# Bucketed attention before two feed-forward layers: sign bits placed under the features of the second score product, scores kept under a ceiling, and copies and loads in another order

## What is computed

```python
q_bits = einsum('bhsd,dk->bhsk', q, proj) > 0          # six bits a token
k_bits = einsum('bhsd,dk->bhsk', k, proj) > 0
mask = bucket(q_bits)[:, :, :, None] == bucket(k_bits)[:, :, None, :]
scores = where(mask, scale * q @ k.T, -1e9)
attn = exp(scores - max(scores)); attn /= attn.sum() + 1e-9
x = (attn @ v), heads laid side by side                # 1536 x 512
x = elu(x @ moe_w_in) @ moe_w_out                      # 512 -> 2048 -> 512
out = (s * relu(x @ moe2_w_in)**2 + b) @ moe2_w_out    # 512 -> 2048 -> 512
```

## Time and profile before

| | us |
|---|---|
| three runs | 781.66, 784.97, 785.71 (median 784.97) |
| the profiled execution | 782.37 |
| its span | 780.6 |
| PE busy (matmul) | 763.5 (98%), 3800 instructions |
| PEld busy (weight loads) | 644.7 (83%) |
| DVE busy (VectorE) | 405.1 (52%) |
| ACT busy (ScalarE) | 343.6 (44%) |
| POOL busy (GpSimd) | 288.9 (37%) |

### The profile page before, as it was taken

One profiled execution on the slowest core, in us unless ns is written; L12 is line 12 of the kernel. 1 busy time (PEld: TensorE's weight loads), 2 busy tenths in 40 slices (PEclk: granted clock), 3 DMA queues, 4 the chain that ended last, 5 costly groups with the idle time before them and its releaser, 6 DMA issues.

```text
span 780.6 us, 12163 instructions
## 1 busy us (share of the span) xinstructions
PE 763.5 (98%) x3800; PEld 644.7 (83%) x3800; DVE 405.1 (52%) x688; ACT 343.6 (44%) x657; POOL 288.9 (37%) x230
## 2 busy tenths in 40 slices
PE   7999999999999999999999999999999999999998
PEld 6788888888889888888888888888888888888886
DVE  5888887888898574343333432352323333242333
ACT  7988898888987221232212322132221312222121
POOL 3688878878897493000000366660000000000000
PEclk9999999999999999999999999999999999999999
DMA  6576667666762342000000032310001000010001
GB/s 168 136 148 167 146 141 177 151 127 157 157 120 61 84 136 82 1 0 1 1 0 1 27 100 89 107 55 0 1 1 42 11 0 0 0 54 0 0 0 54
DMA packets 46312, 52.77 MB, mean 68 GB/s; under 512 B 8912, under 2 KB 34768, under 8 KB 46288
## 3 DMA queue, kind: packets, MB, share of 16 engines
q1 hardware_dynamic: 46064, 52.13, 27.0%
q10 hardware_dynamic: 224, 0.33, 0.2%
HBM read 32.73 MB, written 3.19 MB: 46 GB/s over the span
## 4 chain that ended last, share of the span: by engine, by line
PE 75%; DMA 8%; POOL 6%; issue 5%; SPq 3%; DVE 2%; ACT 0%; POOLq 0%; DVEq 0%
PE acc L594 33%; PE h_ps L576 32%; DMA inv_dram<-row_inv 4%; DMA all_inv<-inv_dram 3%; PE pt_ps L542 2%; POOL wa_lo L431 2%; POOL kt L385 2%; PE pv_ps L556 2%; PE pv_ps L557 1%; PE s_ps L528 1%; PE s_ps L529 1%; POOL wa_hi L429 1%; POOL pt_hi L395 1%; DMA w_raw<-w_out_dram 1%; DVE w_raw L837 1%
## 5 line engine op out<-in xcount | busy, mean ns | idle before, releaser
L770 ACT ACTIVATE r_sb<-h_ps 128x512 f32<-128x512 f32 x96 | 57.4, 598 | 368.0 <-PE h_ps L576 368.0
L909 DVE TENSOR_SCALAR g_sb<-e_sb,sb_scale 128x512 f32<-128x512 f32 x48 | 27.9, 582 | 158.2 <-ACT e_sb L773 158.2
L907 DVE SCALAR_TENSOR_TENSOR g_sb<-e_sb,h_ps 128x512 f32<-128x512 f32 x48 | 33.0, 687 | 135.6 <-ACT e_sb L773 135.1
L804 DVE TENSOR_REDUCE row_min<-s_ps 128x1 f32<-128x768 f32 x96 | 91.5, 954 | 10.3 <-PE s_ps L529 9.6
L693 ACT ACTIVATE probs<-s_ps,row_min 128x768 f32<-128x768 f32 x96 | 87.0, 906 | 11.3 <-DVE row_min L804 9.3
L542 PE MATMUL pt_ps<-cst,probs 128*128 128x128 f32 x576 | 80.8, 275 | 0.7 <-DVE pt_lo L811 0.5
L556 PE MATMUL pv_ps<-pt_hi,v_nat 128*128 128x384 f32 x192 | 72.6, 378 | 7.8 <-DVE w_raw L837 7.7
L576 PE MATMUL h_ps<-xt_hi,wa_lo 128*128 (+1 forms) x192 | 74.7, 389 | 0.0
L576 PE MATMUL h_ps<-xt_lo,wa_hi 128*128 (+1 forms) x192 | 74.7, 389 | 0.0
L576 PE MATMUL h_ps<-xt_hi,wa_hi 128*128 (+1 forms) x192 | 74.7, 389 | 0.0
L576 PE MATMUL h_ps<-xt_hi,wb_hi 128*128 (+1 forms) x192 | 74.7, 389 | 0.0
(11 more groups left out here) (93 smaller groups left out, 1598.3 us busy)
## 6 DMA issues: line engine op xcount, KB each, us to landing
qt<-kt SPq DMA_DIRECT2D x45, 192.0 KB, 3.0
w_raw<-w_in_dram SPq DMA_DIRECT2D x32, 256.0 KB, 2.7
w_raw<-w_out_dram SPq DMA_DIRECT2D x32, 256.0 KB, 2.9
all_inv<-inv_dram SPq DMA_DIRECT2D x32, 192.0 KB, 3.7
raw<-qk_dram SPq DMA_DIRECT2D x15, 384.0 KB, 4.3
raw_v<-v_dram SPq DMA_DIRECT2D x16, 192.0 KB, 4.7
out_dram<-o_sb SPq DMA_DIRECT2D x12, 256.0 KB, 2.1
kt<-kt SPq DMA_DIRECT2D x15, 192.0 KB, 3.7
```

What stands on the lines that cost most here:

```text
L804: nc.vector.tensor_reduce(row_min[:, k:k + 1], s_ps[k % 2][:, :, 0:HALF], AX.XY, ALU.min).then_inc(min_done, 1)
```

## The change

The mask moves into 12 rows under the 64 features of the second product. For each of six bits there is a row for "bit set" and one for "bit clear"; q's rows hold +2^31 for its own side, k's rows -2^31 for the other, so each differing bit adds -2^62 to q·k. VectorE writes scores times -SCALE, under a ceiling of 2^56, to SBUF and takes the row's minimum in the same instruction; the exponential works in place there. The product of counts, the one-hot, the penalty and the scaling of q fall away. All sign products of a head stand in unit 5, the bits are written in unit 0 and one DMA lays them under q and k.

In `scores`, `exp` and the keeping of scores:

```diff
-                wait(pe, exp_done, u - 1)
+                wait(pe, scores_kept, u - 1)
-                q2 = qt2[par][:, t * P:(t + 1) * P]
+                q2 = qt2[par][score_rows, t * P:(t + 1) * P]
...
-                    last = mm(s_ps[buf][:, n, 0:HALF], q2, kt2[par][:, cols], start=False, stop=True)
+                    last = mm(s_ps[buf][:, n, 0:HALF], q2, kt2[par][score_rows, cols], start=False, stop=True)
...
-            def row_minimum(u, k):
+            def keep_scores(u, k):
                 dve.wait_ge(scores_done, u + 1)
-                nc.vector.tensor_reduce(row_min[:, k:k + 1], s_ps[k % 2][:, :, 0:HALF], AX.XY,
-                                        ALU.min).then_inc(min_done, 1)
+                wait(dve, pt_done, 2 * u - 2 * (SRING - 1))
+                ts(probs[k % SRING][:].rearrange("p (n c) -> p n c", n=2), s_ps[k % 2][:, :, 0:HALF], -SCALE, CEILING,
+                   ALU.mult, ALU.min, accum_out=row_min[:, k:k + 1]).then_inc(scores_kept, 1)
...
-                act.wait_ge(min_done, u + 1)
-                wait(act, pt_done, 2 * u - 2)
-                nc.scalar.activation(probs[k % 2][:].rearrange("p (n c) -> p n c", n=2), s_ps[k % 2][:, :, 0:HALF],
-                                     ACT.Exp, bias=row_min[:, k:k + 1], scale=-1.0,
-                                     accum_out=row_sum[:, k, 0:1]).then_inc(exp_done, 1)
+                act.wait_ge(scores_kept, u + 1)
+                scores = probs[k % SRING]
+                nc.scalar.activation(scores[:], scores[:], ACT.Exp, bias=row_min[:, k:k + 1], scale=-1.0,
+                                     accum_out=row_sum[:, k:k + 1]).then_inc(exp_done, 1)
```

Bits, the copies of q and of the bits, and the move of x of second heads (SRING is 3; `bit_rows` are partitions 64 to 75, `score_rows` 0 to 75; the sign products now give 48 rows):

```diff
+            def to_bits(dst, z, rows, thr, amp):
+                return ts(dst, z, planes_in_sb[rows, thr:thr + 1], planes_in_sb[rows, amp:amp + 1], ALU.is_gt, ALU.mult)
+
+            def copy_q_hi(head, par):
+                sp.wait_ge(qk_hi, head)
+                sp.dma_start(qqk[par][top, 0:2, :].bitcast(F32),
+                             hi.unsqueeze(1).to_broadcast([DH, 2, SEQ])).then_inc(q_hi_copied, 16)
...
+            def copy_bits(head, par):
+                sp.wait_ge(bits_done, head)
+                sp.nop(nofuse=True)
+                sp.wait_ge(q_lo_copied, 16 * head)
+                sp.dma_start(qqk[par][bit_rows, 1:3, :].bitcast(F32), bits[:].bitcast(F32)).then_inc(bits_copied, 16)
...
-                sp.dma_start(x_other[n][low, :], x_second[top, :]).then_inc(second_moved[n], 16)
-                sp.dma_start(x_main[n][low, :], x_second[low, :]).then_inc(second_moved[n], 16)
+                sp.dma_start(x_parts[n][low, :, :], x_second[n][:]).then_inc(second_moved[n], 16)
```

`x_second` becomes two buffers, `raw_v` two, x no longer lies in a weight buffer; the parts of v of odd heads are written interleaved, every second column. The order of SP's queue in a pair:

```diff
                 copy_k(2 * i + 1, 1)
+                copy_bits(2 * i + 1, 1)
                 if prev:
+                    get_inv(i, -1)
                     move_second(i - 1, 0)
-                    get_inv(i, -1)
+                if nxt:
+                    load_qk(2 * i + 3, 1)
+                    load_v(2 * i + 2, 0)
                 put_inv(i, 0)
-                load_v(2 * i + 1)
+                get_inv(i, 0)
                 if nxt:
-                    copy_q(2 * i + 2, 0)
+                    copy_q_hi(2 * i + 2, 0)
                 if prev:
                     move_second(i - 1, 1)
-                get_inv(i, 0)
-                if after:
-                    load_qk(2 * i + 4, 0)
                 if nxt:
-                    load_w(0, i + 1, 0, i + 1)
+                    copy_q_lo(2 * i + 2, 0)
                 put_inv(i, 1)
                 if nxt:
                     copy_k(2 * i + 2, 0)
+                    copy_bits(2 * i + 2, 0)
+                get_inv(i, 1)
                 move_first(i, 0)
-                get_inv(i, 1)
+                if after:
+                    load_qk(2 * i + 4, 0)
                 put_inv(i, 2)
...
```

GpSimd adds the epsilon (`add_eps`) and splits weights only in the first and the last pair (EARLY is 4 in place of 8; the other twelve tiles are split beside the first chunk):

```diff
-            def pair(i, prev=True, nxt=True):
+            def pair(i, prev=True, nxt=True, weights=()):
                 split_third(i, 0)
-                split_w(at(wa_hi, i), at(wa_lo, i), i, 0, i + 1)
+                add_eps(i, 0)
+                if weights:
+                    split_w(at(wa_hi, weights[0]), at(wa_lo, weights[0]), weights[0], 0, weights[0] // 2 + 1)
+                if prev:
+                    split_x(i - 1, 0)
                 if nxt:
                     split_qk(2 * i + 2, 0)
+                add_eps(i, 1)
                 split_third(i, 1)
                 if prev:
-                    split_x(i - 1, 0)
+                    split_x(i - 1, 1)
                 split_third(i, 2)
-                split_v(2 * i + 1, 1)
-                if prev:
-                    split_x(i - 1, 1)
+                add_eps(i, 2)
+                split_v(2 * i + 1, 1, i + 1)
+                if weights:
+                    split_w(at(wa_hi, weights[1]), at(wa_lo, weights[1]), weights[1], 1, weights[1] // 2 + 1)
                 if nxt:
                     split_qk(2 * i + 3, 1)
+                add_eps(i, 3)
                 split_third(i, 3)
```

More of the change, by code:

```diff
@@ L461, in _ @@
             split_qk(1, 1)
[L462 to L463 removed]
+            split_v(0, 0, 1)
+            pair(0, prev=False, weights=(0, 1))
             with pool.Fori(1, PAIRS - 1) as i:
                 pair(i)
[L466 removed]
+            pair(PAIRS - 1, nxt=False, weights=(2, 3))
             for n in range(2):
@@ L506, in counts, with first_signs @@
-            def counts(head, n, bank=prep_ps):
-                pe.wait_ge(bits_done, head + 1)
-                rows = slice(n * BIT_ROWS, n * BIT_ROWS + 2 * BITS)
-                mm(bank[:, 0:HALF], code[rows, :], bits[rows, :], start=True, stop=True).then_inc(counts_done, 1)
-            def buckets_out(count):
-                wait(pe, onehot_done, count)
-                wait(pe, penalty_done, count)
+            def first_signs():
+                pe.wait_ge(planes_built, 1)
+                pe.wait_ge(k0_in, 16)
+                pe.wait_ge(q0_in, 16)
+                for n in range(2):
+                    last = mm(s_ps[1][0:HEAD_ROWS, n, 0:HALF], planes0[:].rearrange("p w r -> p (w r)")[:, 0:HEAD_ROWS],
+                              raw[0][:, n * HALF:(n + 1) * HALF], start=True, stop=True)
+                last.then_inc(z0_done, 1)
@@ new lines, in signs @@
+            def signs(head, par):
+                pe.wait_ge(planes_split, 1)
+                pe.wait_ge(qk_split, head)
+                wait(pe, bits_done, head - 1)
+                dst = prep_ps[0:SIGN_ROWS, 0:HALF]
+                for n in range(2):
+                    cols, plane = slice(n * HALF, (n + 1) * HALF), slice(n * SIGN_ROWS, (n + 1) * SIGN_ROWS)
+                    mm(dst, planes_hi[:, plane], kt1[par][:, cols], start=n == 0, stop=False)
+                    mm(dst, planes_lo[:, plane], kt1[par][:, cols], start=False, stop=False)
+                    last = mm(dst, planes_hi[:, plane], kt2[par][:, cols], start=False, stop=n == 1)
+                last.then_inc(z_done, 1)
@@ L613, in unit @@
                 transpose_probs(i, u, k, 1)
-                if follows and t == CODE_A:
-                    counts(head, 0)
-                if follows and t == CODE_B:
-                    buckets_out(2 * head + 1)
-                    counts(head, 1)
                 if third == 0 and not (first and k < 2 * HT):
@@ new lines, in _ @@
+            laid, sign = [planes_in_sb[:, c:c + 2 * BIT_PAIR].rearrange("p (w r) -> p w r", w=2) for c in (C_PROJ, C_SIGN)]
+            tt(planes0[:, :, 0:BIT_PAIR], laid, sign, ALU.mult).then_inc(planes_built, 1)
+            for n in range(2):
+                tt(planes[:, n, :, :, n].rearrange("p r w -> p w r"), laid, sign, ALU.mult).then_inc(planes_built, 1)
+            dve.wait_ge(k0_hi, 1)
+            tt(kt2[0][top, :], raw[0][top, :], kt1[0][top, :].bitcast(F32), ALU.subtract).then_inc(k0_lo, 1)
```

428 lines of the change are left out of this document (194 added, 234 removed).

## The result

The changed kernel takes 789.65 us (median of seven runs, 788.68 to 794.61), the kernel before beside it 782.38 (781.17 to 785.71). The ratio is 1.0092, with a 95% interval of 1.0062 to 1.0122. The forecast was 767.0 with a range of 757 to 778 and a chance of 0.88 for faster; it was wrong in its sign, and the measured time lies outside the range. The profiled execution took 788.98 us for a span of 787.2, 6.6 above the span of before.

The account below looks back on a forecast made before the run. In attention no engine bounds alone; TensorE, VectorE, ScalarE and GpSimd are nearly equally full, and TensorE fills the feed-forward layers. Gains 12.4 + 1.4 + 0 + 2.5 = 16.3 from 782.4 give 766.1, plus 0.9: 767 us, range 757 to 778.

Parts of the forecast that it names:

- the middle pairs: Six pairs of attention heads between pair 0 and the last: 28.4 us each against 30.46, 12.4 in all.
- The work taken away: Attention: four count products leave TensorE per pair, 0.46 us each, 1.84 in all; TensorE's own time becomes 26.8 a pair.
- plain beat: Time between first transposes of successive attention units without signs or counts: 2.05 us, forecast 2.05 to 2.2.
- VectorE's excess: Units 0 to 2 of each head: VectorE's 6.6 us load against TensorE's 6.15, costing 1.0 us a pair.
- The scores' minimum: VectorE keeps scores and takes their row minimum in one instruction: 0.95 us plus 0.1 for the minimum's output.
- SP's queue: DMA issue in attention: inverses' put-and-fetch path needs 8.0 of 8.4 us, bits' copy hidden; 0.3 us of waits a pair.
- GpSimd's queue: GpSimd's work in attention falls from 25.1 to 22.4 us a pair; 0.3 for v of the odd head, ready just in time.
- Last pair and pair 0: Last pair gains 0, between +1.5 and -2, because GpSimd splits two weights there; pair 0 gains 1.4 us.
- Start: Before the first transposes: they begin at 11.7 us instead of 14.17, 2.5 less, between 1.5 and 3.5.
- GpSimd holds everybody: Rival: in attention GpSimd's load becomes 31 us a pair, VectorE's reciprocal waits for its add; slower, 789 us; chance 0.10.
- The fetch is the new bound: Rival: VectorE or the factors' fetch bounds attention, 1.5 us of DMA waits, pairs of 29.8; 777 us; chance 0.18.

Follow-up runs that it names:

- e9: e7 with the second weight tile loaded after pair 0's first fetch and the first split by GpSimd behind pair 0's second third; 766.57 us, ratio 0.9767.
- e6: The changed kernel with two lines moved in SP's queue, so q's upper copies go ahead of the fetches of the factors; 775.79 us, ratio 0.9894.
- e1: The changed kernel with GpSimd's additions of x back behind the second third and behind v; 786.99 us, ratio 1.0052.
- e5: The changed kernel with both e1's order of GpSimd and e6's order of SP; 772.15 us, ratio 0.9841.
- e2: The kernel before with only GpSimd's additions of x placed early as in the change; 792.13 us, ratio 1.0116.
- e7: e5 with the weight loads spread one by one over pair 0 and the middles of pairs 6 and 7; 772.41 us, ratio 0.9862.
- e3: The changed kernel with epsilon added by VectorE ahead of its reciprocal instead of by GpSimd; 792.93 us, ratio 1.0105.
- e10: The changed kernel with a second buffer for the raw thirds (pt_raw); 792.08 us, ratio 1.0104.
- e11: e6 with a second buffer for the raw thirds (pt_raw); 777.13 us, ratio 0.9905.
- e12: e6 with GpSimd's split of q and k ahead of the first addition of x; 779.43 us, ratio 0.9956.
- e4: The changed kernel with GpSimd adding second-head x to itself, so VectorE instead of GpSimd waits for the move's DMA; 785.34 us, ratio 1.0021.

## Why the prediction was wrong, point by point

The forecast added up 12.4 for the middle pairs, 1.4 for pair 0, 0 for the last pair and 2.5 for the start, 16.3 us won. The profiled execution has -3.4, +1.0, -4.8 and +0.6, 6.6 lost.

**The work taken away: right.** A count and its company cost 0.46 of the beat, and the plain beat is 2.07 to 2.08 in the changed kernel. Once the queues are in order a middle pair takes 27.88 (e9), against a forecast of 28.4 and TensorE's own 26.8. The product over 76 rows has the duration of one over 128 (343 ns each), as taken. The weights that are now split beside the first chunk are hidden, as forecast: with e9's order the last part is 554.3 for 554.1.

**VectorE's excess: not borne out.** The difference of 27.88 to 26.8, 1.1, is near the 1.0 that the forecast gave VectorE, but by luck. That 1.0 was to lie in units 0 to 2 of each head, and there the beats of e9 are 2.07 to 2.18. What is left in e9 is 0.66 in the beat from unit 10 to 11, by GpSimd's addition of x; the rest is a plain beat of 2.07 for 2.05, sign beats of 3.29 and 3.14 for about 3.1, and 0.1 at unit 2.

**The scores' minimum: right.** 957 and 85 ns make 1.04. The Trainium skill ("VectorE: DVE Perf Modes", "Two Vector instructions with no wait between them") has it as two instructions, and the rows show both.

**SP's queue: the step that failed most.** The prediction said "Now the fetch of group 0 follows its put", left 0.3 us a pair for waits because the path to the normalisation fits, and held the copy of the bits to be hidden. It asked when the fetched factors are needed, and not what stands behind a fetch that can only be issued when its put has landed, 3.8 us after issue. In the kernel before q's copies were in that gap (put at 110.78, fetch at 118.45), and I read these 7.7 us as a loss of the old order; they were its cover. The three copies of q in it:

```profile
114.52 0.48 SPq L256 DMA_DIRECT2D qt<-kt  x1
115.04 0.59 SPq L257 DMA_DIRECT2D qt<-kt  x1
116.44 0.46 SPq L259 DMA_DIRECT2D qt<-kt  x1
```

The forecast named the queue behind SP's wait for the bits but not behind this one. Cost: 2.2 us a middle pair (31.02 to 28.85 with two lines moved, e6), 2.0% in all by the ratios (1.0092 to 0.9894). Nor do the queues carry less, as the prediction had it: the DMA share in 126 to 155 us is 0.66 as before.

**GpSimd's queue: the second.** The step counted GpSimd's work (22.4 us, under TensorE's 26.8) and gave 0.3 for deadlines, with v of the odd head as the tightest. The two tighter ones are the split of q and k, for which the next head's signs wait, and the second third, for which ScalarE's copy waits through the one `pt_raw`. Both stand behind an addition that waits for a DMA. A sum of work under the bound says nothing of an in-order queue with such a wait in its middle. Cost: 1.2 us a middle pair with SP's order as changed (e1), 0.8 with it mended (e6 to e5), 1.5 in the kernel before (e2).

**Last pair and pair 0: the term was mis-sized.** The last pair got 0, between +1.5 and -2, from GpSimd's load. It lost 4.8 us, not by GpSimd's work but by a beat of 6.8, in which the scores waited 3.87 us for sign bits issued behind 1 MB of weights. SP's and GpSimd's orders give 1.7 of it back (557.2 in e5), and e7's spread loads the other 2.9 (554.3), with the same splits. That each load of weights also is in front of something on the DMA engines was not in the sum.

**Start: partly right.** Transposes from 11.7 were forecast; the experiments with the same start have them from 11.45 to 13.70, the changed kernel at 13.59. The missed 1.9 us of the changed kernel are two: VectorE began the first bits at 7.66 where 6.7 was estimated for the sign products, and a subtraction for which the prediction had at most 0.5 us took 1.54 (below). The early starts won nothing, they lost: in e3, e5, e6, e10 and e11 pair 0 then takes 34.1 to 34.2 us, waiting for its bits behind the weights, where the late starts have 28.6 to 28.7, so pair 1 begins 3.4 to 3.9 us later.

**The rivals.** "GpSimd holds everybody" ended at 789 and the measurement is 789.65, but that is luck: the wait of VectorE's reciprocal for GpSimd's add is there, and taking the add away won nothing (e3). "The fetch is the new bound" had the right place at the wrong price, 1.5 us of waits a pair, and not the right victim. The pair of 27.88 and the time of 766.57 in e9 say that the forecast was one for a kernel whose queues are in order. That e9 meets the 767 so closely is in part luck: its middle pairs are 3 us in all below the forecast, and its start and pair 0 together 3.5 above.

## What to carry to other kernels

When a change moves entries of an in-order queue, write for each entry that waits on a transfer what stands behind it and when that is due; a sum of work per engine doesn't show this. A transfer that must follow another's landing goes behind whatever else can be issued in between. When one wait falls, look for the next one behind the same entry before calling the first one the cause: a second buffer (e10, e11) took a wait of 22 to 32 us away, a swap (e12) one of 6.5 us of TensorE itself, and neither won anything.

## What the hardware showed unexpectedly

**VectorE and GpSimd in each other's way.** The subtraction that splits the planes at the start (two SBUF inputs, 96 columns) took 1.54 us in the changed kernel, where one of 88 columns took 0.25 before. VectorE's and GpSimd's timelines:

```profile
10.05 1.54 DVE L880 TENSOR_TENSOR planes_lo<-planes,planes_hi 128x96 fp32r<-128x96 f32 x1
...
9.65 1.82 POOL L404 TENSOR_TENSOR qqk<-raw,kt 128x768 fp32r<-128x768 f32 x1 [1.09 <-ACT kt L712]
```

It begins after GpSimd's subtraction and ends beside it, at 11.6 and 11.5. In the nine other kernels with this start in which it came first it took 0.26, and transposes began at 11.45 to 12.28; where it came second it took 1.70 and 1.80 (e12, e4) and they began at 13.70 and 13.44. The Trainium skill says the same ("SBUF — State Buffer", "Who interferes with whom"): a VectorE instruction with two SBUF inputs contends with a GpSimd instruction that reads SBUF. The prediction cited that section for the kept scores, which have one input and were not slowed, and not for this instruction.

**The clock adds to a stall.** At the start of the changed kernel TensorE waits 1.40 us for the kept scores, which stand behind that subtraction (0.45 in e6). The mean granted clock of 12.0 to 17.5 us is then 0.71, and the first beat is 3.85; e6 has 1.00 and 2.46.

```profile
12.62 0.42 PE L561 MATMUL s_ps<-kt,qqk 128*128 128x384 f32 x1 [1.40 <-DVE probs L815]
...
12.00:17.50 5.50, 4.86 (x21) 3.87 (x22) 2.98 (x7) 3.61 (x8) 3.08 (x3) 0.71 0.93 244
```

In the last pair of the changed kernel TensorE stood 3.87 us, and the products after it come 0.32 us apart instead of 0.17. The granted clock from 239.90 is half, the level of 1.2 GHz:

```profile
239.94 0.66 PE L561 MATMUL s_ps<-kt,qqk 128*128 128x384 f32 x1 [3.87 <-DMA qqk<-bits]
240.40 0.52 PE L562 MATMUL s_ps<-qqk 76*128 76x384 f32 x1
240.72 0.52 PE L561 MATMUL s_ps<-kt,qqk 128*128 128x384 f32 x1
...
239.90:242.50 2.60, 2.56 (x11) 2.50 (x11) 1.50 (x3) 0.26 (x1) 0.37 (x1) 0.50 0.16 12
243.50:246.00 2.50, 2.50 (x19) 2.47 (x18) 2.02 (x5) 2.01 (x5) 2.27 (x4) 1.00 0.74 156
```

So a wait of 3.9 us made a beat of 6.82, 4.75 over the plain one. Over a whole execution the changed kernel was granted 0.987 to 0.996 of the full clock in its seven runs, the kernel before, in the runs beside the experiments, 0.998 to 1.000. As an estimate, from that difference times the span, this takes 2 to 10 us of TensorE's full speed away, as much as the whole loss. How much of it fell where TensorE stood anyway, and cost nothing, isn't separated.

**Open.** Why pairs 0 with an early start wait longer for their bits than the start is earlier is known only in part: with the weights out of the way (e7, e9) the start is early and the beat at unit 3 has no stall, but with the weights in front the late starts have none either. e12's twelve runs spread from 776 to 782 us, and the spread goes with the clock: the seven granted 0.995 or more took 776.1 to 780.1, the five at 0.991 to 0.993 took 780.1 to 782.4. Whether those five had more stalls or a lower clock first, no trace shows.
